# Expert tiles of 208 tokens with the weights stationary, in a fused attention, mixture-of-experts and MLP kernel

## What is computed

```python
# stage 2: N, D, E, F = 1536, 512, 8, 1024
logits = x @ w_gate
e_idx = np.argmax(logits, axis=1)
...
for e in range(E):
    mask = e_idx == e
    h = np.maximum(x[mask] @ w1[e], 0.0)
    ye = h @ w2[e]
    out[mask] = gate_w[mask, None] * eom[mask, e, None] * ye
# stage 3: d_ff = 2048
h = x @ w_in
g = h * (1.0 / (1.0 + np.exp(-1.702 * h)))
return g @ w_out
```

## Time and profile before

| | us |
|---|---|
| median of 3 runs | 767.47 |
| lowest, highest | 765.41, 767.53 |
| the profiled execution | 768.05 |
| its span, first to last instruction | 766.3 |
| PE busy | 737.4 (96%) |
| DVE busy | 423.2 (55%) |
| ACT busy | 375.9 (49%) |
| attention ends, about | 276 |
| first `down` of expert 0's second tile begins | 304.05 |
| first `dense_down` of the MLP begins | 501.48 |

### The profile page before, as it was taken

One profiled execution on the slowest core, in us unless ns is written; L12 is line 12 of the kernel. 1 busy time (PEld: TensorE's weight loads), 2 busy tenths in 40 slices (PEclk: granted clock), 3 DMA queues, 4 the chain that ended last, 5 costly groups with the idle time before them and its releaser, 6 DMA issues.

```text
span 766.3 us, 11526 instructions
## 1 busy us (share of the span) xinstructions
PE 737.4 (96%) x4013; PEld 626.9 (82%) x4013; DVE 423.2 (55%) x789; ACT 375.9 (49%) x721; POOL 168.6 (22%) x249
## 2 busy tenths in 40 slices
PE   7899999999999998899999999999999999999995
PEld 5688999988899976688888888788888888888884
DVE  5678798888878876656565656444222212121211
ACT  3777887887877953655656565533011101011110
POOL 5324424344864950000000000004202000020002
PEclk9999999999999998999999999999999999999998
DMA  7885374553737156856455633330001000010001
GB/s 151 198 188 124 76 166 109 117 126 86 189 95 238 63 193 219 304 193 243 144 176 195 232 140 123 124 110 1 0 1 56 0 1 1 0 56 1 0 1 55
DMA packets 60157, 86.13 MB, mean 112 GB/s; under 512 B 31552, under 2 KB 33600, under 8 KB 59584
## 3 DMA queue, kind: packets, MB, share of 16 engines
q1 hardware_dynamic: 53872, 74.69, 33.6%
q0 software_dynamic: 2352, 6.31, 2.2%
q10 hardware_dynamic: 3872, 4.36, 1.8%
HBM read 55.97 MB, written 8.92 MB: 85 GB/s over the span
## 4 chain that ended last, share of the span: by engine, by line
PE 80%; DVE 5%; SPq 4%; DMA 3%; POOL 3%; issue 2%; ACT 1%; ACTq 1%; DVEq 0%; POOLq 0%
PE ps L1024 17%; PE ps L727 11%; PE ps L806 6%; PE ps L1039 6%; PE ps L1041 6%; PE ps L1040 6%; PE ps L940 4%; PE ps L942 3%; PE ps L941 3%; PE ps L953 3%; PE ps L955 3%; PE ps L954 3%; SPq L413 3%; PE ps L782 3%; PE ps L778 3%; PE ps L793 2%
## 5 line engine op out<-in xcount | busy, mean ns | idle before, releaser
L1305 ACT ACTIVATE g<-ps 128x512 f32<-128x512 f32 x48 | 28.7, 598 | 205.4 <-PE ps L1024 203.3
L1706 DVE CAST gt_h<-g 128x512 fp32r<-128x512 f32 x48 | 21.0, 438 | 179.0 <-ACT g L1305 175.1
L1435 DVE TENSOR_TENSOR pt_l<-ps,pt_h 128x384 fp32r<-128x384 f32 x192 | 98.0, 551 | 32.7 <-ACT pt_h L1132 31.6
L1391 DVE TENSOR_REDUCE nmax<-ps 128x1 f32<-128x768 f32 x96 | 91.0, 948 | 4.9 <-PE ps L782 4.9
L1132 ACT CAST pt_h<-ps 128x384 fp32r<-128x384 f32 x192 | 84.9, 486 | 16.1 <-PE ps L727 16.1
L1108 ACT ACTIVATE probs<-ps,nmax 128x768 f32<-128x768 f32 x96 | 88.3, 920 | 6.4 <-DVE nmax L1391 6.4
L727 PE MATMUL ps<-ident,probs 128*128 128x128 f32 x576 | 83.6, 276 | 2.8 <-ACT probs L1108 1.9
L1024 PE MATMUL ps<-x2t_h,wl 128*128 128x512 f32 x192 | 74.9, 390 | 1.4 <-DVE wl L1616 1.4
L727 PEld LDWEIGHTS ps<-ident,probs 128*128 128x128 f32 x576 | 65.7, 140 | 12.6 <-DVE pt_l L1435 6.6
L1039 PE MATMUL ps<-wh,gt_l 128*128 128x512 f32 x192 | 74.8, 389 | 0.0
L1024 PE MATMUL ps<-x2t_h,wh 128*128 128x512 f32 x192 | 74.7, 389 | 0.0
(11 more groups left out here) (210 smaller groups left out, 1486.0 us busy)
## 6 DMA issues: line engine op xcount, KB each, us to landing
raw<-in_moe_w SPq DMA_DIRECT2D x32, 1024.0 KB, 6.9
ka<-hi_t SPq DMA_DIRECT2D x32, 192.0 KB, 4.2
raw<-in_moe_w_in SPq DMA_DIRECT2D x4, 1024.0 KB, 5.7
raw<-in_moe_w_out SPq DMA_DIRECT2D x4, 1024.0 KB, 6.6
xg<-xs ACTq DMA_DIRECT2D x15, 256.0 KB, 3.4
qn<-in_q SPq DMA_DIRECT2D x16, 192.0 KB, 3.7
vn<-in_v SPq DMA_DIRECT2D x8, 384.0 KB, 4.5
qa<-hi_t SPq DMA_DIRECT2D x16, 192.0 KB, 3.6
```

Of the source, the lines that this page charges most:

```text
L1391: nc.vector.reduce_max(nmax[:, s % 4:s % 4 + 1], halves(score_bank(s)), AX.XY, negate=True).then_inc(m_ready, 1)
L1435: nc.vector.tensor_tensor(pt_l[g % 2][at_p], ps[:, 4 + half, 0:GQ].rearrange("p (c n) -> p c n", c=GT), pt_h[g % 2][at_p].bitcast(F32), AL ...
```

## The change

Expert 0's first two tiles are done as before. For all others the roles of the operands are exchanged: **a tile is 208 tokens (`WIDE`), the weights are stationary and the tokens move**, in both layers.

- `wide_transpose`: 8 transposes of 104x128 turn two halves of 104 tokens (`xg` now holds 104 x 2 x 512).
- `wide_hidden`: for each of 8 blocks of 128 hidden values, 12 matmuls of 208 columns into bank f % 4; the result already has hidden values on partitions. ScalarE writes `relu` of it as `hw_h` (`wide_relu`), VectorE `hw_l` (`wide_low`), each of 208 columns. No hidden transposes.
- `wide_down`: for each of the 8 blocks, 12 matmuls of 208 columns into banks 4 to 7; the result is turned already, and `wide_out` and `wide_out_low` write it into `x2t_h` and `x2t_l` (4 x 208 columns each). No `y32`, no `turned`.

With the counts above there are 8 such tiles: one for each of experts 1 to 6, two for expert 7, none for expert 0. Each costs TensorE 192 matmuls of 208 columns and 8 transposes. A tile's `down` now follows its own `hidden`; only the transposes of the next tile stand between its matmuls. The whole of an expert's splits (8 on each engine) lies in its first tile, and for expert 7 four more, of the MLP's `w_in`. The last tile is finished before the MLP begins. `fill` copies 208 rows of zeros from DRAM to DRAM, and those of experts 1 and 2 are issued behind the load of expert 0's second tile.

```diff
+    WIDE = 208
+    HW = WIDE // 2
+    LEAD = WIDE - TILE
...
-                sp.dma_start(xs[bass.ds(n + e * REGION, TILE), :], zeros[:, :]).then_inc(s_pad[e], 16)
-
+                sp.dma_start(xs[bass.ds(n + e * REGION, WIDE), :], xs[E * REGION:E * REGION + WIDE, :]).then_inc(s_pad[e], 16)
...
-            for e in range(3):
-                fill(e)
+            fill(0)
             sp.wait_ge(s_pad[0], 16)
             sp.wait_ge(s_disp, 16 * NT)
-            sp.dma_start(xg[:, :], xs[TILE:2 * TILE, :]).then_inc(xg_in, 16)
+            sp.dma_start(xg[:, 0, :], xs[TILE:2 * TILE, :]).then_inc(xg_in, 16)
+            fill(1)
...
+            def wide_hidden(g, e, f):
+
+                slot = 2 * (e % 2)
+                if f >= 4:
+                    pe.wait_ge(hwl_done, FC * g + f - 3)
+                first = True
+                for c in range(DC):
+                    if f == 0:
+                        pe.wait_ge(w1_lo if e else w0_lo, 4 * (e - 1 if e else 0) + c + 1)
+                    w = slice(c * FE + f * P, c * FE + (f + 1) * P)
+                    for a, b in ((wl, xt_h), (wh, xt_l), (wh, xt_h)):
+                        last = nc.tensor.matmul(ps[:, f % 4, 0:WIDE], a[slot][:, w], b[:, c, :], start=first, stop=(c == DC - 1 and a is wh and b is xt_h))
+                        first = False
+                last.then_inc(hidden_done if f == FC - 1 else hw_ready, 1)
...
+            def expert_tile(g, e, k):
+
                 pe.wait_ge(xtl_done, g + 1)
-                hidden(g, e, 0)
-                down(p, ep, 4)
-                down(p, ep, 6)
-                hidden(g, e, 1, 0, 2)
-                hidden_transpose(g, 0)
-                turned(p)
-                hidden(g, e, 1, 2)
...
+                for f in range(FC):
+                    wide_hidden(g, e, f)
+                pe.wait_ge(x2l_done, g + 1)
+                wide_down(g, e, 0)
+                wide_down(g, e, 1)
+                pe.wait_ge(hwl_done, FC * g + FC)
+                wide_transpose(g + 1)
+                for f in range(2, FC):
+                    wide_down(g, e, f)
...
+            def wide_out(g, row):
+
+                act.wait_ge(y_ready, g + 1)
+                nc.scalar.copy(x2t_h[:, :, bass.ds(row, WIDE)], ps[:, 4:8, 0:WIDE]).then_inc(x2h_done, 1)
...
+                for f in range(FC):
+                    wide_relu(g, f)
+                    if k == 0 and f % 2:
+                        split_second(e, f // 2)
+                wide_tile_high(g + 1)
+                if k == 0:
+                    for i in range(4):
+                        split_first(e + 1, i)
+                    if e == E - 1:
+                        for i in (0, 2, 1, 3):
+                            split_second(E, i)
+                wide_out(g, row)
```

More of the change, by code:

```diff
@@ L222, in clustered_attention_moe_mlp @@
         gt_l = [ml(f"gt_l{i}", [P, 512], F32R) for i in range(2)]
-        ob = [zeros] + [ml(f"ob{i}", [P, DM]) for i in range(1, 4)]
+        ob = [ml(f"ob{i}", [P, DM]) for i in range(4)]
         mlp.close()
@@ L355, in score_bank, with expert_loop @@
             return 2 * (s % 2)
-        def expert_loop(eng, counter, tile, only=None, alike=False):
+        def expert_loop(eng, counter, tile):
             for e in range(E):
@@ L363, in expert_loop @@
                     eng.reg_add(counter, counter, 1)
-                    if only is not None:
-                        with eng.If(n < 2):
-                            only(e)
-                if e and not alike:
-                    with eng.If(n > 1):
-                        tile(eng.snap(counter), e, 1)
-                        eng.reg_add(counter, counter, 1)
-                done = 1 if e and alike else 2
+                done = 1 if e else 2
                 with eng.If(n > done):
                     with eng.Fori(done, n):
-                        tile(eng.snap(counter), e, 2)
+                        tile(eng.snap(counter), e, 1)
                         eng.reg_add(counter, counter, 1)
@@ L983, in _, with wide_transpose @@
             hidden(1, 0, 1, 2)
+            def wide_transpose(t):
+                pe.wait_ge(xg_in, 16 * t + 16)
+                for c in range(DC):
+                    for h in range(2):
+                        at_c = (c % 2) * WIDE + h * HW
+                        last = nc.tensor.transpose(ps[:, 2 + c // 2, at_c:at_c + HW], xg[0:HW, h, c * P:(c + 1) * P], ident[0:HW, 0:HW])
+                last.then_inc(xt_ready, 1)
+            down(1, 0, 0)
+            hidden_transpose(1, 1)
+            down(1, 0, 2)
@@ L1005, in _ @@
-            expert_loop(pe, tiles, expert_tile, alike=True)
-            last = pe.snap(tiles)
-            total = last + 1
-            down(last, E - 1, 0)
-            tile_transpose(total)
-            down(last, E - 1, 2)
-            hidden_transpose(last, 1)
+            pe.reg_mov(tiles, 2)
+            def wide_hidden(g, e, f):
[3 more added lines that the diff above has]
+                first = True
+                for c in range(DC):
+                    if f == 0:
[5 more added lines that the diff above has]
+                last.then_inc(hidden_done if f == FC - 1 else hw_ready, 1)
@@ new lines, in wide_down @@
+            def wide_down(g, e, f):
+                slot = 2 * (e % 2) + 1
+                if f >= 4:
+                    pe.wait_ge(hwl_done, FC * g + f + 1)
+                if f % 2 == 0:
+                    pe.wait_ge(w2_lo if e else w0_lo, 4 * (e - 1 if e else 1) + f // 2 + 1)
+                for c in range(DC):
+                    w = slice(f * DM + c * P, f * DM + (c + 1) * P)
+                    for a, b in ((wl, hw_h), (wh, hw_l), (wh, hw_h)):
+                        first = f == 0 and a is wl
+                        last = nc.tensor.matmul(ps[:, 4 + c, 0:WIDE], a[slot][:, w], b[:, f, :], start=first, stop=(f == FC - 1 and a is wh and b is hw_h))
+                if f == FC - 1:
+                    last.then_inc(y_ready, 1)
@@ L1708, in _ @@
                     nc.vector.tensor_tensor(gt_l[f % 2][:, :], g32[f % 2][:, :], gt_h[f % 2][:, :].bitcast(F32), ALU.subtract).then_inc(g2_done, 1)
-                    if m == 0 and f == 1:
-                        turned_low(last, row, 3)
                     if m == 0 and f < 8:
```

267 lines of the change are left out of this document (133 added, 134 removed).

## The result

| | before | after |
|---|---|---|
| median, us | 766.44 | 795.57 |
| lowest, highest | 765.09, 767.53 | 793.84, 797.78 |
| span of the profiled execution | 766.3 | 794.4 |
| ratio of the medians | | 1.037 [1.034, 1.040] |

The change makes the kernel 29 us slower; 763.7 was predicted, within 752 to 786. The time is lost in two places. Between the first `down` of expert 0's second tile and the first `dense_down` lie 222.36 us instead of the 197.4 of the earlier trace rows, and from there to the last matmul of high by low (the third last of the kernel) 259.35 instead of 255.10, in code that the change doesn't touch. The way up to that first `down` is 1.1 us shorter: 24.9 + 4.25 - 1.1 = 28.05, the difference of the spans but for rounding.

A forecast was written before the change was run, and what follows sets the result against it. TensorE was taken to bound the stretch: 190.2 us of matmuls and transposes plus 3.5 of waits, 193.7 instead of 197.4. That is -3.7 us, from the median 767.47 to 763.7, range 752 to 786.

The forecast's parts named there:

- The matmul, 0.111 us: Wide products: each pair of weight load and 208-column matmul is bound by the load, 0.111 us; 1536 take 170.5 us.
- Rivals 1, 2 and 4: Wide matmuls: stream binds, 748 to 759 (0.12); instruction supply binds, 785 (0.12); narrow fp32r at fp32's rate, 1108 (0.03).
- rival 2: Wide products: TensorE's instruction supply can't keep 0.111 us per pair; at 0.125 the time is 785 us; chance 0.12.
- the two figures that the prediction quotes against this term: Wide products: the skill's times per matmul of 128 and 512 columns, estimated near 93 ns for 208, 143 us for 1536.
- The sum of the stretch: Rewritten stretch, 304.05 to 501.45 us before: 190.2 of TensorE work plus 3.5 of waits, 193.7 instead of 197.4 us.
- the turning: Expert 0's second tile: wait between the last down and the transposes of its copied result, 0.9 us.
- expert 7's second tile: There wide_relu and wide_low, delayed by splits and the loop's edge, end too late for block 4: 1.0 us.
- the join to the MLP: Before the MLP: the first split of w_out stands behind the first activation, 6.0 us against 5.4 of two dense: 0.6.
- Seven boundaries between tiles, a slow start of 0.1 each: 0.7: Between wide tiles: TensorE was to lose only a slow start at each of seven boundaries, 0.7 us together.
- Rival 3: TensorE's loop edge: the queue covers half as long; 1 us showing at each of 7 boundaries gives 771; chance 0.08.
- Costed at nothing: Weight transfers, longer xg loads, small ScalarE and VectorE instructions ahead of the loop, and fills: taken as adding 0 us.
- rival 5: Tile count: a token count just over 208 adds one tile, 22 us, giving 786; chance 0.03 together with others.

The follow-up runs named there:

- e7: e1 with each wide matmul streaming only 104 of the 208 columns, all weight loads kept; 766.95 us.
- e1: Changed kernel with tile numbers fixed in TensorE's program, so no count read, branch or skipped body there; 766.51 us.
- e14: Changed kernel; on TensorE one loop from 0 to the count for experts 1 to 7, expert 0's skip hinted, its and expert 1's counts read earlier; 766.94 us.
- e13: e1 with rows of x2t_h and x2t_l of 6656 bytes instead of 6976; 762.12 us.
- e6: Changed kernel; TensorE's skipped body for experts 0 to 6 holds only wide_hidden, 96 matmuls and 96 loads; 770.69 us.
- e11: Kernel before, with TensorE's skipped body four tiles long for experts 0 and 1; 784.04 us.
- e12: Changed kernel with a hint naming the target ahead of every skipping branch of TensorE; 773.29 us.
- e2: Changed kernel; TensorE's skipped body for experts 0 to 6 holds only a register addition; 769.70 us.

## Why the prediction was wrong

- **The matmul, 0.111 us: right.** Measured 8.05 / 72 = 0.112, at full clock, and not bound by the stream (e7). The 0.11 of the earlier trace rows, from pairs of loads, held over 1536 of them. Rivals 1, 2 and 4 were about this number, and all three are out. That TensorE can be fed at this pace was the doubt of rival 2: e1 keeps it for 177 us without a gap. (A straight line through the two figures that the prediction quotes against this term, 81 and 131 ns, gives 91 for 208 columns and not its 93; it was in no sum.)
- **The sum of the stretch: right but for the control flow.** 193.7 predicted, 192.2 in e1, 193.0 in e14, 191.8 in e13. The waits were 0.68 at the turning (0.9), none in expert 7's second tile (1.0; at 497.07 its 96 matmuls take 10.72) and 0.5 at the join to the MLP (0.6).
- **The failed step: "Seven boundaries between tiles, a slow start of 0.1 each: 0.7".** It took the boundary's price from the kernel before, where the skipped body was 128 instructions and only experts 0 and 1 skipped theirs. Measured are 13.1 us of idle time at the boundaries and just behind them, 8.6 at the entry and some 9 of half clock behind: 30 us (222.4 against the 192.2 of e1), of which 0.7 was in the sum. What they are is TensorE waiting for the instructions behind a skipped body of 400. Rival 3 named the place, "the loop's edge on TensorE", with 1 us at each boundary and a chance of 0.08. Its mechanism, a queue that covers half as long, was not the one: with a body of 96 matmuls and the same queue no boundary shows (e6), and the old kernel with long bodies loses 17 us (e11). Its size was a quarter of the loss.
- **The entry was in no term.** The listing ahead of the prediction has the register read and the branch between the last transposes of `y` and the first wide product. The sum had 0.9 us for the turning there and nothing for what the branch jumps over. The 8.6 us of idle time there are the largest single loss.
- **"Costed at nothing" left out the MLP.** Its code is the same, and so the sum passed over it; its operand's rows are not the same. 4.25 us, more than the gain forecast.
- **The range** reached to 786 for rival 2 and rival 5. The time lies 10 us beyond, since the two causes were in no rival at their size.

What the profile of before could have told: the profile's page counts a queue of instruction fetches, with 33 packets of 16 KB. How many instructions a skipped body has on each engine, before and after (128 and 400), is counted from the code. Neither was looked at.

## What to carry to other kernels

Before a loop body grows, count its instructions on each engine where the loop may be skipped: here a skip over 192 cost nothing more than a skip over one, while one over 400 mostly cost 2.5 us (once 1.2, once nothing), or 8.6 beside 1 MB transfers, and then up to 2.5 us of half clock. Write such a loop so that the usual case runs through it (from 0 to the count), and hint the branches that have to stay. When a buffer's row length changes, time what reads it too: from 6656 bytes to 6976, or only to 6720, the MLP lost 4.2 us.

## What the runs showed of the hardware

- A taken branch over 400 TensorE instructions cost 2.4 to 2.6 us at four of six boundaries, with the DMA engines 0.37 to 0.50 busy, and 8.3 to 8.6 at the entry, at 0.93 in the changed kernel; over 512 instructions it cost 3.5 at 0.68 and 10.2 at 0.96 (e11); over 192 or fewer nothing beyond the 1.5 us of a register read and branch on a short queue. A hint took the changed kernel's 21.7 us of idle time to 3.9.
- Where one packet of 16 KB of instructions was missing, TensorE's next matmul started 3.3 to 3.6 us after the packet did (seven gaps, and the entry's of e12); the packet itself is listed with 0.9 to 1.4 us.
- Idle time of PE of 1.5 (e2) to 10.2 us (e11) was followed by stretches of 4 to 5 us at a mean granted clock of 0.50 to 0.68 (the lower level is 0.50, 1.2 GHz), worth 1.6 to 2.5 us on matmuls of 0.111, but not each time: behind the 2.57 us at 371.08 there was none (47 matmuls in 5.47 us), and behind e14's 0.94 none.
- Pairs of a 128x128 fp32r weight load and a matmul start 0.111 to 0.112 us apart with 208 columns and with 104; eight transposes with loads of 104 rows 0.09 apart. The Trainium skill ("TensorE: Matmul & The Clock Gate", section "Back-to-back issue gap") has 81 ns for 128 columns; no row here reaches it.
- A moving operand in rows of 6656 bytes streams 512 columns in 226.7 ns whichever row it is; in rows of 6720, 6784 or 6976 bytes rows 1 to 3 take 224 to 241, 231 (6784) to 235 on average, and row 0 stays at 227.
